# Expert stage of a fused attention and mixture kernel: another table for the weight chunks, last tile out of the loop, a row buffer of its own for tile 1

## The reference

```python
def _moe2_ref(x, w_gate, w1, w2):              # the stage that is changed
    logits = x @ w_gate
    expert_idx = np.argmax(logits, axis=1)
    ...                                        # gate_w: softmax probability of the chosen expert
    for e in range(E):
        mask = expert_idx == e
        h = np.maximum(x[mask] @ w1[e], 0.0)
        out[mask] = gate_w[mask, None] * (h @ w2[e])

def reference(**kwargs):
    attn_out = _attn_ref(**attn_kwargs)        # linear attention: 8 batches, 8 heads, 576 x 64
    x = attn_out as 4608 rows of 512
    x = _moe_ref(x=x, **moe_kwargs)            # ((x @ w1) * (x @ w2)) @ w3 @ w_out
    return _moe2_ref(x=x, **moe2_kwargs)       # 8 experts, 512 -> 1024 -> 512, one expert per token
```

## Time and profile before

| | us |
|---|---|
| median of 3 runs | 1526.4 (1525.47 to 1526.71) |
| the profiled execution, its own time | 1525.93 |
| its span | 1524.2 |
| PE busy | 1475.9 (97%) |
| DVE, ACT, POOL busy | 996.9, 722.6, 621.9 |
| expert stage in the loop, from the profile | about 1057.5 to 1512.6 |

### The profile page before, as it was taken

How to read it: one execution, slowest core, us unless ns; L and a number is a source line. 1 busy time by engine, 2 the same in 40 slices (tenths; PEclk the granted TensorE clock), 3 DMA queues, 4 the chain that set the end, 5 groups by cost and what they waited for, 6 DMA issues and landing times.

```text
span 1524.2 us, 28767 instructions
## 1 busy us (share of the span) xinstructions
PE 1475.9 (97%) x8066; PEld 1275.8 (84%) x8067; DVE 996.9 (65%) x1881; ACT 722.6 (47%) x1555; POOL 621.9 (41%) x649
## 2 busy tenths in 40 slices
PE   7999999999999999999999999999999789999995
PEld 6999999999978888888888888887888668888884
DVE  5688888888826374564746556335788567877663
ACT  4688787887712222122221212144666456675551
POOL 5676676766810012020210202113676485664221
PEclk9999999999999999999999999999999899999998
DMA  6354344435330202022020211136333243311110
GB/s 246 118 140 113 99 106 110 105 100 137 93 119 1 83 1 83 22 61 62 21 83 0 83 28 55 35 137 214 123 129 142 97 156 110 129 38 54 40 48 30
DMA packets 84760, 135.19 MB, mean 89 GB/s; under 512 B 50048, under 2 KB 50304, under 8 KB 80498
## 3 DMA queue, kind: packets, MB, share of 16 engines
q1 hardware_dynamic: 76978, 114.01, 24.7%
q0 software_dynamic: 7744, 20.69, 4.2%
HBM read 104.78 MB, written 30.94 MB: 89 GB/s over the span
## 4 chain that ended last, share of the span: by engine, by line
PE 66%; POOL 1%; issue 1%; DVE 1%; ACT 1%; DMA 1%; POOLq 0%; ACTq 0%; DVEq 0%
PE bank L164 64%; POOL big L1083 1%; PE bank L1620 1%; DMA out<-arena,ids 1%; ACT arena L1220 1%; DVE xs L1436 0%; DVE arena L1421 0%; ACT big L807 0%; PE bank L1551 0%; DVE xs L1400 0%; PE bank L1559 0%; PE bank L1570 0%; PE bank L1651 0%; PE bank L1545 0%; ACTq L821 0%
## 5 line engine op out<-in xcount | busy, mean ns | idle before, releaser
L164 PE MATMUL bank<-big,xs 128*128 (+1 forms) x2112 | 500.7, 396 | 30.4 <-DVE xs L1436 10.2
L164 PEld LDWEIGHTS bank<-big,xs 128*128 128x128 f32 x2112 | 398.5, 190 | 115.1 <-issue 30.4
L164 PE MATMUL bank<-xs,big 128*128 128x512 f32 x1728 | 397.3, 391 | 2.7 <-PEq L213 2.7
L164 PEld LDWEIGHTS bank<-xs,big 128*128 128x128 f32 x1728 | 324.7, 188 | 70.2 <-issue 2.9
L164 PE MATMUL bank<-big 128*128 128x512 f32 (+1 forms) x1632 | 324.7, 347 | 2.0 <-POOL big L303 1.4
L164 PEld LDWEIGHTS bank<-big 128*128 128x128 f32 (+1 forms) x1632 | 254.7, 164 | 36.2 <-POOL big L303 1.7
L1008 POOL TENSOR_TENSOR arena<-arena 128x512 f32<-128x512 f32 x32 | 37.9, 1194 | 441.0 <-DMA arena<-rec_scratch 441.0
L1369 DVE TENSOR_TENSOR arena<-arena,bank 128x512 f32<-128x512 f32 x72 | 49.4, 686 | 245.1 <-PE bank L164 245.1
L1136 ACT COPY arena<-bank 128x512 f32<-128x512 f32 x72 | 42.3, 587 | 306.3 <-PE bank L164 306.3
L1421 DVE TENSOR_SCALAR arena<-bank,gate 32x256 f32<-32x256 f32 x296 | 142.8, 482 | 46.1 <-PE bank L164 41.0
L1294 DVE CUSTOM_DVE_ANT_0 arena<-arena 128x512 f32<-128x512 f32 x256 | 159.5, 688 | 13.7 <-ACT arena L1156 13.4
(11 more groups left out here) (162 smaller groups left out, 1402.5 us busy)
## 6 DMA issues: line engine op xcount, KB each, us to landing
arena<-we SPq DMA_DIRECT2D x32, 1024.0 KB, 4.9
kqraw<-kq SPq DMA_DIRECT2D x32, 576.0 KB, 3.8
rows_scratch<-arena SPq DMA_DIRECT2D x36, 256.5 KB, 4.9
xT_scratch<-arena SPq DMA_DIRECT2D x32, 288.0 KB
arena<-v SPq DMA_DIRECT2D x64, 128.0 KB, 2.4
arena<-xT_scratch SPq DMA_DIRECT2D x8, 1024.0 KB, 5.5
arena<-rec_scratch SPq DMA_DIRECT2D x64, 128.0 KB, 3.9
arena<-w3T SPq DMA_DIRECT2D x8, 512.0 KB, 3.2
```

Of the source, the lines that this page charges most:

```text
L164: ins = nc.tensor.matmul(out, left[a], right[b], start=first and n == 0, stop=last and n == 2)
```

## The change

It has three parts. The table `CH` is worked out in quarters of an expert with other rules: fewer chunks in the first tile of an expert, and more ahead of a short expert. The last tile is taken out of the loop on all engines. There ACT alone does relu on 128 rows, PE turns the block in the middle of `second_product(38)`, the split block goes to a buffer `htlast` in the arena, and the last result goes to a bank and an output buffer of its own. Tile 1 gets a row buffer of its own, `xt1`; its split is moved forward on ACT and DVE, and on PE the turning of tile 0's block is moved between the two halves of `first_product(1)`.

```diff
+    m["xt1"] = xs[:, :, DM + FF:2 * DM + FF]
+    over("htlast", [2, FF], arena_at, F32R)
...
-        def tiles(eng, body):
-            n = table(m, eng, T, 0, E - 1 + FIRST, TMAX)
+        def tiles(eng, body, left=1):
+            n = table(m, eng, T, left, E - 1 + FIRST - left, TMAX - left)
             with eng.Fori(FIRST, n) as g:
                 body(g)
-            return table(m, eng, T, 1, E - 2 + FIRST, TMAX - 1)
+            return last_of(eng)
...
+            last = tiles(pool, period, 2)
+            last1, last2 = last_of(pool, 1), last_of(pool, 2)
+            tile_chunks(pool, last1, weights)
+            written(last2)
+            scatter(last2)
+            tile_chunks(pool, last, weights)
+            written(last1)
+            scatter(last1)
+            pool.wait_ge(gathered, 16 * last + 16)
+            scatter(last, ylast, m["idg"])
...
             relu_half(0, 0)
+            rows_high(1, False)
             exponents(NB - 1)
             relu_half(0, 1)
-            rows_high(1)
+            next_gate(1)
             h_high(0)
...
-            tiles(act, tile)
+            last = tiles(act, tile)
+            relu(last)
+            tile_chunks(act, last, weights)
+            h_high(last)
...
             choices(NB - 1)
+            rows_low(1)
             gates(NB - 1)
...
-            linked(dve.tensor_scalar(tabf[:, 2], tabf[:, 2], 1.0, float(CPE), ALU.add, ALU.min), base)
...
+            linked(dve.tensor_scalar(ch, ch, 1.0 / CPE, 1.0, ALU.mult, ALU.min), base)
+            linked(dve.scalar_tensor_tensor(ch, ch, 1.0, ex, ALU.add, ALU.add), base)
...
+            last = tiles(dve, tile)
+            for h in range(2):
+                h_low(last, h)
+            result(last_of(dve, 1))
+            dve.wait_ge(y_mm, last + 1)
+            dve.tensor_copy(ylast, ylast_ps[:]).then_inc(y_sb, 1)
...
+            first_product(1, 0, 0, 0)
             h_transpose(0)
-            for h in range(2):
-                first_product(1, h, 0, 0)
+            first_product(1, 1, 0, 0)
...
-            last_tile = tiles(pe, tile)
-            second_product(last_tile, *weights_of(last_tile))
+            g = tiles(pe, tile)
+            g1 = last_of(pe, 1)
+            here, before = weights_of(g), weights_of(g1)
+            for h in range(2):
+                first_product(g, h, *here)
+            second_product(g1, *before, between=lambda: h_transpose(g))
+            second_product(g, *here, out=ylast_ps, left=htlast)
```

More of the change, by code:

```diff
@@ L890, in stage2, with rows @@
         ahead = m["ahead"]
-        xt, ht = m["xt"].rearrange("p s (c n) -> p s c n", c=DC), m["ht"].rearrange("p s (j n) -> p s j n", j=FC)
+        ht = m["ht"].rearrange("p s (j n) -> p s j n", j=FC)
+        xts = [m[name].rearrange("p s (c n) -> p s c n", c=DC) for name in ("xt", "xt1")]
+        def rows(g):
+            return xts[1 if isinstance(g, int) and g == 1 else 0]
         xg, hs, ysb = m["xg"], m["hs"], m["ysb"]
@@ L1038, in gather, with scatter @@
                                         ).then_inc(gathered, 16)
-            def scatter(g):
+            def scatter(g, src=ysb, ids=m["ids"]):
                 row = table(m, pool, ROW, g, 0, E * TPE)
-                pool.tensor_copy(m["ids"][:], m["idall"][:, ds(row, 1)]).then_inc(ids_set, 1)
+                pool.tensor_copy(ids[:], m["idall"][:, ds(row, 1)]).then_inc(ids_set, 1)
                 pool.wait_ge(ids_set, g)
@@ L1178, in rows_high @@
                     act.copy(m["gate"][:], xg[:, DM:XW]).then_inc(gate_set, 1)
-                act.copy(xt[:, 0], xtr_ps[:].rearrange("p (c n) -> p c n", c=DC)).then_inc(xt_hi, 1)
+                act.copy(rows(g)[:, 0], xtr_ps[:].rearrange("p (c n) -> p c n", c=DC)).then_inc(xt_hi, 1)
                 if gate_first:
@@ L1206, in h_high @@
             def h_high(g):
-                if not (isinstance(g, int) and g == 0):
+                late = not isinstance(g, int)
+                if late:
+                    act.wait_ge(w_lo, NCH)
+                elif g > 0:
                     act.wait_ge(y_mm, g)
                 for h in range(2):
-                    act.wait_ge(htr_mm, 2 * g + h + 1)
-                    act.copy(ht[:, 0, h * DC:(h + 1) * DC],
+                    act.wait_ge(htr_mm, 2 * (FIRST if late else g) + h + 1)
+                    act.copy((htlast if late else ht)[:, 0, h * DC:(h + 1) * DC],
                              htr_ps[h][:].rearrange("p (c n) -> p c n", c=DC)).then_inc(ht_hi, 1)
@@ L1399, in rows_low @@
                 dve.wait_ge(xt_hi, g + 1)
-                dve.tensor_tensor(xt[:, 1], xtr_ps[:].rearrange("p (c n) -> p c n", c=DC),
-                                  xt[:, 0].bitcast(F32), ALU.subtract).then_inc(xt_lo, 1)
+                dve.tensor_tensor(rows(g)[:, 1], xtr_ps[:].rearrange("p (c n) -> p c n", c=DC),
+                                  rows(g)[:, 0].bitcast(F32), ALU.subtract).then_inc(xt_lo, 1)
             def result(g):
@@ new lines, in _ @@
+            linked(dve.scalar_tensor_tensor(ch[:, 1:last_g], ahead_of[:, 1:last_g], 2.0,
+                                            ch[:, 1:last_g], ALU.add, ALU.min), base)
+            linked(dve.scalar_tensor_tensor(ch[:, 2:last_g], ahead_of[:, 1:last_g - 1], 2.0 + 2.0 / CPE,
+                                            ch[:, 2:last_g], ALU.add, ALU.min), base)
+            linked(dve.scalar_tensor_tensor(ch[:, 0:last_g], ex[:, 1:last_g + 1], early_w2,
+                                            ch[:, 0:last_g], ALU.add, ALU.max), base)
@@ L1630, in first_product, with second_product @@
                         between()
-                    last = split3(nc, h_ps[h][:], parts(xt[:, :, c]),
+                    last = split3(nc, h_ps[h][:], parts(rows(g)[:, :, c]),
                                   parts(ring[:, :, ds(base + (c * FF + h * HF), HF)]), c == 0, c == DC - 1)
                 last.then_inc(h_mm, 1)
-            def second_product(g, e, base):
+            def second_product(g, e, base, between=None, out=y_ps, left=ht):
                 pe.wait_ge(w_lo, CPE * e + CPE)
-                pe.wait_ge(y_sb, g + 1)
+                if out is y_ps:
+                    pe.wait_ge(y_sb, g + 1)
                 for j in range(FC):
+                    if j == DC and between is not None:
+                        between()
                     if j % DC == 0:
                         pe.wait_ge(ht_lo, 2 * g + j // DC + 1)
-                    last = split3(nc, y_ps[:], parts(ht[:, :, j]),
+                    last = split3(nc, out[:], parts(left[:, :, j]),
                                   parts(ring[:, :, ds(base + (W1C * CW + j * DM), DM)]), j == 0, j == FC - 1)
```

38 lines of the change are left out of this document (19 added, 19 removed).

## The result

The changed kernel takes 1509.18 us (median of 4 runs, 1507.93 to 1511.2) against 1526.27 for the one before: ratio 0.989, 95% interval 0.9873 to 0.9907. The forecast was 1509.3. The profiled execution took 1508.43, with a span of 1506.7 against 1524.2, 17.5 less.

| stretch on PE | before | changed | difference | forecast |
|---|---|---|---|---|
| up to the expert stage's first matmul | 1019.53 | 1019.38 | -0.2 | 0 |
| to the transposes of tile 3's rows (term A) | 31.13 | 30.01 | -1.1 | -1.4 |
| to those of tile 14 (term B) | 127.81 | 126.38 | -1.4 | -0.6 |
| to those of tile 19 (term C) | 76.75 | 69.15 | -7.6 | -8.2 |
| to those of tile 39 | 227.51 | 227.27 | -0.2 | 0 |

What follows compares the result with a forecast made beforehand. PE, busy 97% of the span, bounds the kernel, so only its idle and slow stretches can be won. Terms -1.4 - 0.6 - 8.2 - 6.6 = -16.8 us gave 1509.1 to 1509.6, stated as 1509.3; 8-in-10 range 1504.5 to 1514.5.

Steps and rivals of the forecast that it cites:

- term A: Tile 1's rows: PE's idle 1.43 us goes as DVE splits the rows earlier; -1.4 us (bounds 0 and -1.43).
- term B: Tile 4: PE's lateness of 0.42 + 0.20 us goes with one chunk in tile 3; -0.6 us (0 to -0.62).
- term C: Tiles 12 to 17, new chunk table: 19.1 us lost before, 10.9 after; -8.2 us.
- C1: Tile 13: PE late behind DVE's low part of the turned block, held by a POOL chunk; 3.6 us (1.1 to 9.1).
- C3: Tile 15: PE waits for POOL's two chunks for expert 4's second product; 4.1 us (3 to 4.5).
- C4: Slow clock on PE behind the wait of C3; 1.6 us (0 to 2.9).
- C2: Behind C1, PE's clock drops or PE catches up with the next gather; 1.6 us (1 to 2.9).
- the rule that spoke against the change: VectorE ops with two SBUF inputs and GpSimd ops reading SBUF exclude each other for a whole instruction.
- The first rival: Tiles 12 and 13: two chunks cost little, port merely shared, C1 of 1.1; 1506.2 us, chance 0.20.
- Term D: Last tile out of the loop: no idle time or slow clock, last matmul at 1506.0; -6.6 us (-5.5 to -6.7).
- Chunks of tile 13 late for expert 4: Rival: late chunks hold expert 4's first product, most of term C is spent; 1517.5 us, chance 0.12.
- First products held up at each new expert: Rival, slower: first tiles of experts 1, 2, 5, 6, 7 wait, 11.6 us each; 1532.8 us, chance 0.04.

Runs made afterwards that it cites:

- rows_only: The kernel before with part one alone: tile 1's own row buffer and its split moved forward; 1526.46 us, ratio 0.999.
- rows_gate: rows_only with the gather of tile 2 released when tile 1's gate is saved, not when it is in use; 1524.58 us.
- table_only: The kernel before with the new chunk table alone, ten table ops in place of six; 1518.8 us.
- half_wait: The changed kernel with the second product's wait for its two chunks parted, one at the start, the other at its middle; 1509.12 us.
- low_psum: The changed kernel with DVE's low part made by two 512-column ops, second input a PSUM bank, so other numbers result; 1507.25 us.
- low_two: The changed kernel with DVE's low-part op parted into two 512-column ops, both inputs in SBUF (control for low_psum); 1511.85 us.
- last_only: The kernel before with the last tile out of the loop and nothing else; 1519.12 us.
- spread_table: The changed kernel with seven more DVE table ops, spreading chunks ahead of the short expert so only tiles 13 and 15 have two; 1504.64 us.

## Why the prediction came true, point by point

**The total** came out within 0.2 us of the forecast, and that is luck, where single executions of the changed kernel differ by 3.3 us. Of the stretches, A (-1.1 for -1.4) and C (-7.6 for -8.2) gave less than forecast, and B (-1.4 for -0.6), the tail and the stretches that were set at nothing gave more, and these errors cancel.

**Term A was mis-sized.** The step "the idle 1.43 us goes, I take -1.4" is wrong. The profile gave 1.1, and with part one alone S1 gained nothing (31.15 against 31.13). I had checked the store, the chunk loads and the table behind the moved work, but not the gather of tile 2, which is issued at the same time as before while PE comes 1.4 us earlier; it was in no row I showed, because in the trace of before nobody waited for it. rows_gate shows that it is the cause. The sum also takes it that so short an idle stretch costs no clock, from the one of 1.77 us in the earlier trace rows. That held in the trace of before, but in table_only the idle time of tile 1 was followed by 1.56 us of slow matmuls.

**Term B** was -1.4 and not -0.6 over that stretch. The named waits of 0.42 and 0.20 are in no row of the changed kernel, though PE still starts 0.3 us late once in their place, behind the transposes at 1073.19. Over these two tiles 0.8 us went. The other 0.6 lies further on up to tile 14, where every other tile of the kernel before ran 0.15 to 0.3 us late and those of the changed kernel run at the smooth pace. table_only has the same stretch (126.33 us), so it is the table's gain; I have not tried what held those tiles.

**Term C** was worked out in four pieces, and three of them were met nearly to the digit: C1 3.57 + 0.19 against 3.6, C3 4.10 against 4.1, C4 1.4 against 1.6. C2, the slow clock behind the first wait, was 2.4 against 1.6, within its bounds, and the size of that slow stretch differs between executions of the same tile (1.4 us in table_only, 1.6 in half_wait). That the low part of the block would be held up by a chunk was the rule that spoke against the change, and low_psum and low_two show that it is the mechanism. The first rival (C1 of 1.1) falls with it: beside a chunk the op took 4.09 us. That rival was also priced too low in its own terms. By the forecast's clock PE would then be at expert 4's first product at about 1196.9, with the chunk ready at 1198.4; low_psum, where C1 is nearly gone, shows just such a wait of 1.24 us, and one of 1.46 for the gather that C2 names.

**Term D** was met: 23.3 us from tile 39's transposes, no gap at the loop's exit. last_only shows that it is this part's own gain. The tail became 0.4 us shorter, which I had set at nothing.

**The rivals.** Chunks of tile 13 late for expert 4: not seen in the changed kernel, PE waited for nothing there; as low_psum shows, this is because the wait of 3.57 us ahead of it gives POOL the time. First products held up at each new expert: not seen, from tile 19 on both kernels run the smooth pace (227.5 and 227.3 us). The forecast's argument against it, each expert's second chunk three tiles ahead of its first tile, misreads the table for experts 2 and 4, which have it two tiles ahead (tiles 7 and 13); that was enough too.

## What to carry to other kernels

When a stall is taken out, list everything that PE meets in the next few microseconds and when each of it was issued, also what nobody waits for now: the trace of before shows no wait where there was a margin of a microsecond. Where GpSimd works through long SBUF ops, keep VectorE ops with two SBUF inputs off the path, or give one input from PSUM, and don't part them: each part may have to wait for a whole GpSimd op. Two chunks of work in one period cost little when the next is empty and nothing waits for the second of them (0.40 us in spread_table). Parting a wait so that the first half needs only the first chunk turned a stall of 4.10 us with slow matmuls behind it into one of 1.36 without.

## What the runs showed of the hardware

- A DVE op with one SBUF input beside a PSUM one was untouched by POOL (1.27 us for two of 512 columns), and POOL gained as well: a pair of chunks took 9.15 us instead of 10.02 to 10.18.
- The first matmuls behind an idle stretch of PE of 2.4 to 4.1 us were slow in every profile (1.4 to 2.5 us lost on 48 matmuls, up to 2.9 on the last 24 of rows_only). Behind 1.1 to 2.2 us none was, but for one: in table_only 0.38 and 1.05 us of idle time cost 1.56. A short idle stretch is mostly, but not always, free of that cost.
- An indirect gather issued while the last rows were being stored landed 6.1 to 7.9 us behind its issue, and PE, which came for it after 5.6, waited 0.49 to 2.23 us; those in the loop landed in 3.4 us at the median.
